# Prefix counts in two halves of 64 rows, and the second half of v loaded in two transfers

## The chip, the cores and the metric

The kernel runs on one core of a Trainium2 chip. The metric is device time in microseconds of one execution. A core has a matrix engine (TensorE, PE in the profile, with its weight loads as PEld), a vector engine (DVE), an activation engine (ACT), a general engine (POOL), and a sync engine (SP) that here does little but issue transfers. Operands lie in an on-chip memory of 128 partitions (rows); results of PE go to PSUM banks.

## The reference

Attention without a softmax, then two mixture-of-experts layers:

```python
scores = (1.0 / S) * np.matmul(z, z.transpose(0, 2, 1))     # z: 4 x 2496 x 64
attn = np.maximum(scores, 0.0) ** 2
x = u * np.matmul(attn, v)                                  # u, v: 4 x 2496 x 256
# first layer: rows with x @ w_skip > 0 go to expert argmax(x @ w_gate) of 8, the others stay
out[do_compute] = xc + gate_w * (np.maximum(xc @ w1[e], 0) @ w2[e])
# second layer: all rows, expert argmax(x @ w_gate + modality_bias[modality_id])
out[mask] = gate_w[mask, None] * (np.maximum(x[mask] @ w1[e], 0) @ w2[e])
```

Inputs are float32. 9984 rows pass through.

## The kernel before, in words

Attention runs in 20 chunks `g` of 512 query columns (448 in the last of each batch), five chunks for each of four batches. Within a chunk, 20 key blocks `k` of 128 rows go by in ten pairs `p`. For a block PE makes scores (`scores`, L1469) in a PSUM bank `pS`, ACT applies relu (L725) and square (L734) into a ring of four buffers `A`, DVE splits the square into a high part `AH` (L1118) and a low part `AL` (L1120), and PE sums `v` times these parts into `pO` (`half_sums`, L1480, and `tail_sums`, L1489), three products for each half of the 256 columns. Scores run three pairs ahead of the sums. All these matrix products are done on 64 rows of the array at a time: two matmuls, one on rows 0 to 63 and one on rows 64 to 127 (`halves`), go out as a pair and write to different banks.

`v` comes in halves of ten blocks. SP loads it into `vraw` (`load_v`, L323), which has room for ten blocks, so the second half may only be loaded over blocks that are split already. The split into `VH` is done by DVE in batch 0 (`v_high`, L1104, in the places that `V_AT`, L1123, gives), by ACT in the later batches (L708); the split into `VL` is done by POOL (`v_low`, L551). Five splits of two blocks each belong to a half. PE waits for `vl_ready` before it sums a pair.

While chunk `g` runs, the finished chunk `g-1` is routed. At p = 3 PE transposes half of its rows and computes the gate logits (`route`); at p = 7 it transposes the other half (`route_rows`, L1532, again as pairs of 64 rows, into `pT` and `pM`) and counts how many rows before each row go to each of 16 groups (`prefixes`, L1559): one matmul of the one-hot table `oh` with the triangle `before` (L1562) and four with `ones` (L1564), in bf16, on all 128 rows. DVE picks the experts (`pick_experts`) and at p = 2 of the next chunk turns the counts into destinations (`place_rows`, L1079), which wait for nothing but `prefix_ready` and ACT's copy of the rows. POOL then scatters the rows to memory by an indirect transfer for each 128 rows (L548).

All orders are written out in the code; each engine runs its list from front to back, and semaphores tie them. After chunk 20 comes a seam: the last two chunks must be placed and scattered before SP may load the first tile `xin` of the first expert layer. The two expert layers follow, which the change leaves alone. Each small DVE step that reads the result of the one before it waits for it (`step`); `ROUTE` is the number of such steps in a chunk.

Of the kernel before, what the change touches and what calls it, by code (L numbers as in the profile page):

```python
# [10 lines left out]
ALU = mybir.AluOpType  # L11
# [4 lines left out]
P = 128  # L16
# [4 lines left out]
KT = -(-S // P)  # L21
# [3 lines left out]
QT = 4  # L25
QW = QT * P
QC = KT // QT
CHUNKS = B * QC
NG = KT // QT
VU = KT // 2  # L30
# [6 lines left out]
ZW = KT * P  # L37
VW = KT * D
VHALF = KT // 2
WP = 4  # L40
GR = 2 * E
TT = 256
# [15 lines left out]
STORED = 64  # L58
MIDDLE = (3, 4, 5, 6, 8)
SPLIT_AT = ((B - 1) * QC + 1, (B - 1) * QC + 2)  # L60
ROUTE = 15


def bass_attention_two_moe(nc, u, v, z, w_skip, w_gate, w1, w2, modality, w_gate2, bias2, w2t, out):
    xs = nc.dram_tensor("token_rows", (GR * CAP + SPARE, ROW), F32, kind="Internal").ap()

    with ExitStack() as ctx:
# [6 lines left out]
        def sem(name):  # L74
            return ctx.enter_context(nc.semaphore(name))
# [83 lines left out]
        pM = pb("pM", [P, 512])  # L159
        prefix = pM[:, 2 * P:2 * P + (QT + 1) * GR].rearrange("p (t n) -> p t n", n=GR)  # L160

        xt_halves = [x[:, 0:2 * KD * H].rearrange("p (t k c) -> p t k c", t=2, k=KD) for x in (pT, pM)]

        stage1 = raw[:, 0:KD * F].rearrange("p (k f) -> p k f", k=KD)
# [37 lines left out]
        v_first_loaded = [sem(f"v_first_loaded{i}") for i in range(2)]  # L202
        z_loaded = [sem(f"z_loaded{i}") for i in range(len(Z_PARTS))]
        v_loaded = sem("v_loaded")
        u_loaded = sem("u_loaded")
        zh_ready = sem("zh_ready")
        zl_ready = sem("zl_ready")
# [104 lines left out]
        def _(sp):  # L312
            with nc.allow_non_contiguous_dma(reason="small tables"):
# [9 lines left out]
                def load_v(b, k0, k1):  # L323

                    vb = v[b, :, :]
                    full, at = min(k1, KT - 1), k0 % VHALF
                    to = vraw[:, at * D:(at + full - k0) * D].rearrange("p (j d) -> p j d", d=D)
                    sp.dma_start(to, vb[k0 * P:full * P, :].rearrange("(j p) d -> p j d", p=P)).then_inc(v_loaded if k0 >= FIRST else v_first_loaded[k0 * 2 // FIRST], 16)
                    if k1 == KT:
                        for r in range(2):  # L330
                            sp.dma_start(vraw[r * H:(r + 1) * H, (VHALF - 1) * D:VHALF * D], vb[full * P:S, :]).then_inc(v_loaded, 16)

# [3 lines left out]
                load_v(0, FIRST // 2, FIRST)  # L336
                load_z(0, 2)
                load_v(0, FIRST, VHALF)
                sp.wait_ge(vl_ready, VU // 2)
                load_v(0, VHALF, KT)  # L340
                sp.wait_ge(zeroed, 1)
                sp.dma_start(wg[:, :, 0:E], w_gate.rearrange("(k p) e -> p k e", p=P)).then_inc(consts_loaded, 16)
                sp.dma_start(wg[:, :, E:E + 1], w_skip.rearrange("(k p o) -> p k o", p=P, o=1)).then_inc(consts_loaded, 16)
# [18 lines left out]
                for b in range(B):  # L362
                    for c in range(QC):
                        load_u(b * QC + c)
                        if c == 0 and b < B - 1:
                            sp.wait_ge(zl_ready, NG * b + NG)
                            sp.wait_ge(vl_ready, VU * b + VU)
                            for part in range(len(Z_PARTS)):
                                load_z(b + 1, part)
                            load_v(b + 1, 0, FIRST // 2)  # L370
                            load_v(b + 1, FIRST // 2, FIRST)
                            load_v(b + 1, FIRST, VHALF)
                        if c == 2 and b < B - 1:
                            sp.wait_ge(vl_ready, VU * b + VU + VU // 2)
                            load_v(b + 1, VHALF, KT)

                for ph in range(2):
                    q = PH[ph]
# [277 lines left out]
        def _(act):  # L656
# [51 lines left out]
            def v_high(b, n):  # L708

                at = 2 * (n % (VU // 2)) * D  # L710
                to = (b % 2) * VW + 2 * n * D
                if 2 * n < FIRST:
                    act.wait_ge(v_first_loaded[n], 16 * b + 16)
                else:
                    act.wait_ge(v_loaded, 64 * b + (16 if 2 * n < VHALF else 64))
                s_.copy(VH[:, to:to + 2 * D], vraw[:, at:at + 2 * D]).then_inc(vh_ready, 1)
# [254 lines left out]
        def _(dve):  # L971
# [107 lines left out]
            def place_rows(idx):  # L1079
# [8 lines left out]
                dve.wait_ge(prefix_ready, idx)  # L1088
                if idx < CHUNKS:
                    dve.wait_ge(xrow_copied, 2 * idx + 2)  # L1090
                step(v_.tensor_tensor(rank[:, :, :], prefix[:, 0:QT, :], base[:, None, :].to_broadcast([P, QT, GR]), ALU.add))
                v_.tensor_tensor(base[:, :], prefix[:, QT, :], base[:, :], ALU.add).then_inc(base_ready, 1)
                step(v_.tensor_tensor(rank[:, :, :], rank[:, :, :], oh[:, 0:QT, :], ALU.mult))
                step(v_.tensor_reduce(dest_f[:, :], rank[:, :, :], AX.X, ALU.add))
                if idx > 1:
# [8 lines left out]
            def v_high(n):  # L1104
                w, at = slice(2 * n * D, 2 * (n + 1) * D), 2 * (n % (VU // 2)) * D
                if 2 * n < FIRST:
                    dve.wait_ge(v_first_loaded[n], 16)
                else:
                    dve.wait_ge(v_loaded, 16 if 2 * n < VHALF else 64)
                v_.tensor_copy(VH[:, w], vraw[:, at:at + 2 * D]).then_inc(vh_ready, 1)  # L1110
# [9 lines left out]
                    v_.tensor_tensor(AL[k % NBUF][:, 0:n], A[k % NA][:, 0:n], AH[k % NBUF][:, 0:n].bitcast(F32),  # L1120
                                     ALU.subtract).then_inc(al_ready, 1)

            V_AT = {0: (1,), 1: (2, 3), 2: (4,), 5: (5, 6), 6: (7,), 7: (8,), 8: (9,)}  # L1123
            final_done = [0]

            def f(ins):
# [319 lines left out]
        def _(pe):  # L1446
# [112 lines left out]
            def prefixes(idx):  # L1559

                pe.wait_ge(onehot_ready, idx)
                t_.matmul(pM[:, 2 * P:2 * P + (QT + 1) * GR], before[:, :], oh[:, :, :].rearrange("p t g -> p (t g)"), start=True, stop=False)  # L1562
                for i in range(QT):
                    last = t_.matmul(prefix[:, i + 1:QT + 1, :], ones[:, :], oh[:, i:i + 1, :].to_broadcast([P, QT - i, GR]),  # L1564
                                     start=False, stop=(i == QT - 1))
                last.then_inc(prefix_ready, 1)

            def scores_of(g, p):
# [285 lines left out]
```

## Time and profile before

| | |
|---|---|
| Median of three runs | 1489.77 us (1489.64 to 1490.29) |
| The profiled execution | 1489.09 us, of which the span from the first to the last instruction is 1487.2 us |
| PE busy | 1464.6 us, 98% of the span |
| DVE, ACT, POOL busy | 1009.1, 779.3, 399.2 us |
| Attention, first chunk to seam | about 11 to 704 us of the span |
| Granted TensorE clock, mean | 0.996 |

Times in rows are microseconds from the start of the span. A matrix operation's duration is longer than the distance to the next one, since they are pipelined: what a stream of them costs is read from the distance of the starts. A busy PE is therefore not a PE at its peak: time in which it empties before a change of form counts as busy.

### The profile page before, as it was taken

Reading aid. Unit: us, or ns where it says so; the run is one execution under the profiler, and the core shown is the slowest. Engines: PE = TensorE matmul, PEld = TensorE weight load, DVE = VectorE, ACT = ScalarE, POOL = GpSimd, SP = SyncE. Lnnn points to the kernel's source line nnn. Section 1 sums busy time; section 2 is a strip of 40 time slices with the busy share of each in tenths; the row PEclk is TensorE's granted clock in tenths of the full one; section 3 lists DMA queues with packets and bytes.
Section 4 is the critical chain, followed back from the end, with each engine's and each line's share of the span. In section 5 each row is a group of like instructions: output and inputs, shape, how many; then the busy total and the mean of one; then the engine's idle time right before and its main releaser. Section 6 shows DMA issues by size and latency. Waiting matters only on the chain.

```text
span 1487.2 us, 34548 instructions
## 1 busy us (share of the span) xinstructions
PE 1464.6 (98%) x11853; PEld 1279.1 (86%) x11853; DVE 1009.1 (68%) x2377; ACT 779.3 (52%) x1542; POOL 399.2 (27%) x379
## 2 busy tenths in 40 slices
PE   8999999999999999999899999999999999999997
PEld 7888988888888898888899999998888888888885
DVE  7989987999889998987666666665333343333332
ACT  6677766777667766765344444444333333333332
POOL 4133322334224332323222222224121221211212
PEclk9999999999999999999999999999999999999999
DMA  5311030211302020021533354322211121111110
GB/s 121 100 40 56 29 101 29 66 43 53 92 31 66 29 87 29 30 87 65 180 104 127 121 192 133 106 97 94 90 44 44 43 69 46 43 44 43 58 44 26
DMA packets 58009, 107.74 MB, mean 72 GB/s; under 512 B 18007, under 2 KB 32354, under 8 KB 57884
## 3 DMA queue, kind: packets, MB, share of 16 engines
q0 software_dynamic: 18464, 58.68, 11.3%
q1 hardware_dynamic: 39420, 47.48, 11.1%
q8 instruction: 68, 1.11, 0.3%
q14 instruction: 57, 0.47, 0.1%
HBM read 75.63 MB, written 32.04 MB: 72 GB/s over the span
## 4 chain that ended last, share of the span: by engine, by line
PE 95%; DMA 1%; issue 1%; DVE 1%; POOL 0%; SPq 0%; ACT 0%; POOLq 0%; ACTq 0%; DVEq 0%
PE pO L1480 33%; PE pS L1737 11%; PE pO L1745 10%; PE pS L1469 9%; PE pO L1680 9%; PE pS L1697 9%; PE pO L1747 5%; PE pM L1737 4%; PE pT L1728 1%; PE pO L1489 1%; PE pT L1627 1%; PE pM L1547 1%; PE pT L1532 1%; PE pO L1609 1%; DMA raw<-in_v_dram 0%
## 5 line engine op out<-in xcount | busy, mean ns | idle before, releaser
L1120 DVE TENSOR_TENSOR AL<-A,AH 128x512 fp32r<-128x512 f32 (+1 forms) x400 | 313.5, 784 | 13.7
L1480 PE MATMUL pO<-AH,VH 64*128 64x512 f32 (+1 forms) x1520 | 297.9, 383 | 2.6 <-POOL VL L555 1.3
L1480 PE MATMUL pO<-AL,VH 64*128 64x512 f32 (+1 forms) x1520 | 297.2, 382 | 0.0
L1480 PE MATMUL pO<-AH,VL 64*128 64x512 f32 (+1 forms) x1520 | 296.8, 381 | 0.0
L725 ACT ACTIVATE R<-pS 128x512 f32<-128x512 f32 (+1 forms) x400 | 213.4, 588 | 157.7 <-PE pS L1469 157.4
L734 ACT ACTIVATE A<-R 128x512 f32<-128x512 f32 (+1 forms) x400 | 229.7, 624 | 11.1 <-DVE AL L1120 10.9
L1118 DVE CAST AH<-A 128x512 fp32r<-128x512 f32 (+1 forms) x400 | 212.9, 532 | 30.9 <-ACT A L734 30.6
L1745 PE MATMUL pO<-VL,AH 128*128 128x512 f32 x640 | 232.2, 400 | 0.0
L1378 DVE SCALAR_TENSOR_TENSOR AL<-pS,AH 128x512 fp32r<-128x512 f32 x120 | 83.0, 692 | 157.2 <-ACT AH L896 157.1
L1747 PE MATMUL pO<-VL,AL 128*128 128x256 f32 x640 | 179.2, 280 | 0.0
L609 POOL DMA_INDIRECT out_dram<-xrow,tok_at x80 | 77.8, 973 | 365.4 <-DVE xrow L1388 352.9
L1480 PEld LDWEIGHTS pO<-AH,VH 64*128 64x128 f32 x1520 | 146.7, 184 | 28.5 <-issue 2.9
L1480 PEld LDWEIGHTS pO<-AL,VH 64*128 64x128 f32 x1520 | 146.8, 184 | 24.3
L1480 PEld LDWEIGHTS pO<-AH,VL 64*128 64x128 f32 x1520 | 146.8, 184 | 23.7
L1737 PE MATMUL pS<-ZH,VH 128*128 (+1 forms) x480 | 161.7, 391 | 0.3 <-issue 0.3
L896 ACT ACTIVATE AH<-pS 128x512 fp32r<-128x512 f32 x120 | 71.7, 598 | 171.0 <-PE pS L1737 170.8
L1745 PEld LDWEIGHTS pO<-VL,AH 128*128 128x128 f32 x640 | 120.2, 188 | 26.4
L567 POOL TENSOR_TENSOR xT<-xT,uT 128x512 f32<-128x512 f32 x38 | 50.2, 1325 | 301.7 <-DVE xT L1021 301.4
L1680 PE MATMUL pO<-ZH,VH 128*128 x736 | 128.3, 286 | 0.5 <-issue 0.5
L1747 PEld LDWEIGHTS pO<-VL,AL 128*128 128x128 f32 x640 | 120.5, 188 | 2.4
L1697 PE MATMUL pS<-VL,AH 128*128 128x264 f32 x736 | 120.8, 286 | 0.0
L855 ACT ACTIVATE AH<-pO 128x512 fp32r<-128x512 f32 x92 | 52.6, 598 | 118.7 <-PE pO L1680 118.7
(249 smaller groups left out, 2493.6 us busy)
## 6 DMA issues: line engine op xcount, KB each, us to landing
raw<-in_w_dram POOLq DMA_DIRECT2D x22, 1024.0 KB, 7.7
A<-token_rows SPq DMA_DIRECT2D x21, 536.0 KB, 3.5
uT<-in_u_dram SPq DMA_DIRECT2D x16, 512.0 KB, 3.7
xin<-token_rows SPq DMA_DIRECT2D x24, 268.0 KB, 3.0
raw<-in_v_dram SPq DMA_DIRECT2D x4, 1152.0 KB, 5.8
A<-in_w2t_dram POOLq DMA_DIRECT2D x8, 512.0 KB, 4.8
raw<-in_v_dram SPq DMA_DIRECT2D x4, 768.0 KB, 7.3
raw<-in_z_dram SPq DMA_DIRECT2D x8, 368.0 KB, 5.0
```

Of the source, the lines that this page charges most:

```text
L725: s_.activation(R[k % 2][:, 0:n], pS[k % 2][:, 0:n], ACT.Relu, scale=1.0 / S).then_inc(relu_done, 1)
L734: s_.activation(A[k % NA][:, 0:n], R[k % 2][:, 0:n], ACT.Square).then_inc(square_done, 1)
L1118: v_.tensor_copy(AH[k % NBUF][:, 0:n], A[k % NA][:, 0:n]).then_inc(ah_ready, 1)
L1120: v_.tensor_tensor(AL[k % NBUF][:, 0:n], A[k % NA][:, 0:n], AH[k % NBUF][:, 0:n].bitcast(F32), ALU.subtract).then_inc(al_ready, 1)
L1378: v_.scalar_tensor_tensor(out=AL[f][:, :], in0=ring[f % RING][:, :], scalar=0.0, in1=AH[f][:, :].bitcast(F32), op0=ALU.max, op1=ALU.subtra ...
L1469: last = t_.matmul(pS[r][:, 0:n], w[rows, (2 * p + r) * P:(2 * p + r + 1) * P], x[rows, zc:zc + n], start=(m == 0), stop=(m == 2))
L1480: last = t_.matmul(pO[:, (KD * r + d) * QW:(KD * r + d) * QW + n], vv[rows, vo + k * D + d * P:vo + k * D + (d + 1) * P], a[k % NBUF][rows ...
L1680: last = t_.matmul(pO[:, bank * 512 + fi * TT:bank * 512 + (fi + 1) * TT], w[h][:, kd, f * P:(f + 1) * P], x[:, ds(par, 1), kd, :].rearran ...
L1697: last = t_.matmul(pS[s][:, 0:width], a[p][:, fi * TT + s * P:fi * TT + (s + 1) * P], w[h][:, f, 0:width], start=(f == 0 and n == 0), stop ...
L1737: last = t_.matmul(ring[f % RING][:, :], w[h][:, kd, f * P:(f + 1) * P], x[:, ds(par, 1), kd, :].rearrange("p o t -> p (o t)"), start=(n = ...
L1745: t_.matmul(pO[:, s * QW:(s + 1) * QW].rearrange("p (m d) -> p m d", m=2), AH[f][:, rows], w2hl[h][:, :, f, 0:D], start=(f == 0), stop=(f ...
L1747: return t_.matmul(pO[:, s * QW:s * QW + D], AL[f][:, rows], w2h[h][:, f, 0:D], start=False, stop=(f == NF - 1), skip_group_check=True)
```

## The change

`prefixes` is done for chunks 1 to 19 as two halves: for rows 0 to 63 into a part of `pT`, for rows 64 to 127 into the same part of `pM`, ten matmuls of 64 rows in place of five of 128. `place_rows` adds both halves, with two more DVE instructions, each a waited step. The last routing (idx 20), after the attention, stays whole. Apart from that, the second half of `v` is loaded as six blocks (10 to 15), which wait for three `VL` splits, and then the other four, which wait for five; a semaphore of their own tells of the six. DVE's splits of v blocks from pair 5 on stand one pair earlier in its list.

```diff
+VMID = VHALF + 6
-ROUTE = 15
+ROUTE = 17
...
+        prefix_halves = [x[:, 2 * P:2 * P + (QT + 1) * GR].rearrange("p (t n) -> p t n", n=GR) for x in (pT, pM)]
...
+                sp.wait_ge(vl_ready, (VMID - VHALF) // 2)
+                load_v(0, VHALF, VMID)
                 sp.wait_ge(vl_ready, VU // 2)
-                load_v(0, VHALF, KT)
+                load_v(0, VMID, KT)
...
                         if c == 2 and b < B - 1:
+                            sp.wait_ge(vl_ready, VU * b + VU + (VMID - VHALF) // 2)
+                            load_v(b + 1, VHALF, VMID)
                             sp.wait_ge(vl_ready, VU * b + VU + VU // 2)
-                            load_v(b + 1, VHALF, KT)
+                            load_v(b + 1, VMID, KT)
...
+                parts = prefix_halves if idx < CHUNKS else [prefix]
+                step(v_.tensor_tensor(rank[:, :, :], parts[0][:, 0:QT, :], base[:, None, :].to_broadcast([P, QT, GR]), ALU.add))
+                if idx < CHUNKS:
+                    step(v_.tensor_tensor(base[:, :], parts[0][:, QT, :], base[:, :], ALU.add))
+                    step(v_.tensor_tensor(rank[:, :, :], parts[1][:, 0:QT, :], rank[:, :, :], ALU.add))
+                v_.tensor_tensor(base[:, :], parts[-1][:, QT, :], base[:, :], ALU.add).then_inc(base_ready, 1)
...
+                elif VHALF <= 2 * n < VMID:
+                    dve.wait_ge(v_mid_loaded, 16)
...
-            V_AT = {0: (1,), 1: (2, 3), 2: (4,), 5: (5, 6), 6: (7,), 7: (8,), 8: (9,)}
+            V_AT = {0: (1,), 1: (2, 3), 2: (4,), 4: (5,), 5: (6, 7), 6: (8,), 7: (9,)}
...
+                parts = list(zip(prefix_halves, halves)) if idx < CHUNKS else whole
+                for to, rows in parts:
+                    t_.matmul(to, before[rows, :], oh[rows, :, :], start=True, stop=False)
                 for i in range(QT):
+                    for to, rows in parts:
+                        last = t_.matmul(to[:, i + 1:QT + 1, :], ones[rows, :], oh[rows, i:i + 1, :].to_broadcast([P // len(parts), QT - i, GR]),
+                                         start=False, stop=(i == QT - 1))
```

PE's list at p = 7 of a chunk, before: the last transposes (L1532), the five matmuls of the count, the next scores (L1469).

```order
L1532 MATMUL pT<-ident,xT 128x64
L1532 MATMUL pM<-ident,xT 128x64
L1562 MATMUL pM<-oh,before 128x80 [waits onehot_ready]
L1564 MATMUL pM<-oh,ones 128x64
L1564 MATMUL pM<-oh,ones 128x48
L1564 MATMUL pM<-oh,ones 128x32
L1564 MATMUL pM<-oh,ones 128x16
L1469 MATMUL pS<-ZH 128x512 [waits relu_done]
```

The same place in the changed kernel, where these lines are L1548, L1581, L1584 and L1485:

```order
L1548 MATMUL pT<-ident,xT 128x64
L1548 MATMUL pM<-ident,xT 128x64
L1581 MATMUL pT<-oh,before 128x80 [waits onehot_ready]
L1581 MATMUL pM<-oh,before 128x80
L1584 MATMUL pT<-oh,ones 128x64
L1584 MATMUL pM<-oh,ones 128x64
L1584 MATMUL pT<-oh,ones 128x48
L1584 MATMUL pM<-oh,ones 128x48
L1584 MATMUL pT<-oh,ones 128x32
L1584 MATMUL pM<-oh,ones 128x32
L1584 MATMUL pT<-oh,ones 128x16
L1584 MATMUL pM<-oh,ones 128x16
```

Each count matmul has become two, one for each half of the rows, side by side like the transposes ahead of them.

DVE's list in chunk 0 from pair 5 on, before (L1118 and L1120 split a block of squares, L1110 two blocks of v):

```order
L1102 TENSOR_TENSOR ZL<-raw,ZH 128x512 [waits zh_ready]
L1118 CAST AH<-A 128x512 [waits pv_done,square_done]
L1120 TENSOR_TENSOR AL<-A,AH 128x512 [waits ah_ready]
L1118 CAST AH<-A 128x512 [waits pv_done,square_done]
L1120 TENSOR_TENSOR AL<-A,AH 128x512 [waits ah_ready]
L1110 CAST VH<-raw 128x512 [waits v_loaded] x2
```

And now (L1134, L1136, L1126):

```order
L1116 TENSOR_TENSOR ZL<-raw,ZH 128x512 [waits zh_ready]
L1126 CAST VH<-raw 128x512 [waits v_mid_loaded]
L1134 CAST AH<-A 128x512 [waits pv_done,square_done]
L1136 TENSOR_TENSOR AL<-A,AH 128x512 [waits ah_ready]
L1134 CAST AH<-A 128x512 [waits pv_done,square_done]
L1136 TENSOR_TENSOR AL<-A,AH 128x512 [waits ah_ready]
L1126 CAST VH<-raw 128x512 [waits v_mid_loaded] x2
```

One v split has moved ahead of the two square splits, and the next two wait for the six-block transfer alone.

DVE's destinations for a chunk, before:

```order
L1091 TENSOR_TENSOR rank<-pM,base 128x64 [waits xrow_copied,prefix_ready]
L1092 TENSOR_TENSOR base<-pM,base 128x16 [waits route_step]
L1093 TENSOR_TENSOR rank<-rank,oh 128x64
L1094 TENSOR_REDUCE dest_f<-rank 128x4 [waits route_step]
L1097 TENSOR_TENSOR dest<-dest_f,invalid 128x4 [waits route_step]
```

And now:

```order
L1102 TENSOR_TENSOR rank<-pT,base 128x64 [waits xrow_copied,prefix_ready]
L1104 TENSOR_TENSOR base<-pT,base 128x16 [waits route_step]
L1105 TENSOR_TENSOR rank<-pM,rank 128x64 [waits route_step]
L1106 TENSOR_TENSOR base<-pM,base 128x16 [waits route_step]
L1107 TENSOR_TENSOR rank<-rank,oh 128x64
L1108 TENSOR_REDUCE dest_f<-rank 128x4 [waits route_step]
L1111 TENSOR_TENSOR dest<-dest_f,invalid 128x4 [waits route_step]
```

Two instructions are added, and two more of them wait for the one ahead.

## Rows read from the trace of the kernel before

**Rows 1.** The page, part 1: busy time, share, instructions of each engine.
```profile
PE 1464.6 (98%) x11853; PEld 1279.1 (86%) x11853; DVE 1009.1 (68%) x2377; ACT 779.3 (52%) x1542; POOL 399.2 (27%) x379
```

**Rows 2.** Waits of PE: line, releaser, us in total, times, longest.
```profile
PE pT L1627 <- DMA xin<-token_rows: 4.6, 1, 4.6
...
PE pO L1480 <- POOL VL L555: 1.3, 1, 1.3
PE pO L1480 <- DVE xT L1021: 1.2, 1, 1.2
```

**Rows 3.** Timeline of PE at the count: start, us, line, operation, [idle].
```profile
113.91 0.21 PE L1532 MATMUL pT<-ident,xT 64*128 64x64 f32 x1
...
114.09 0.22 PE L1532 MATMUL pT<-ident,xT 64*128 64x64 f32 x1
114.09 0.22 PE L1532 MATMUL pM<-ident,xT 64*128 64x64 f32 x1
114.24 0.21 PE L1562 MATMUL pM<-oh,before 128*128 128x80 bf16 x1
114.28 0.26 PE L1564 MATMUL pM<-oh,ones 128*128 128x64 bf16 x4
114.47 0.50 PE L1469 MATMUL pS<-ZH 64*128 64x512 f32 x2
114.81 0.40 PE L1469 MATMUL pS<-ZL,ZH 64*128 64x512 f32 x2
115.04 0.39 PE L1469 MATMUL pS<-ZH,ZL 64*128 64x512 f32 x2
```

**Rows 4.** Instructions of tile pM, 113.8 to 114.6: duration ns min/median/max.
```profile
L1532 PEld LDWEIGHTS pM<-ident,xT x4: 135/138/140, 113.7 to 114.0; 64*128 64x128 f32 x4
...
L1564 PEld LDWEIGHTS pM<-oh,ones x4: 96/98/105, 114.3 to 114.3; 128*128 128x128 bf16 x4
L1564 PE MATMUL pM<-oh,ones x4: 169/182/200, 114.3 to 114.4; 128*128 128x64 bf16 x1, 128*128 128x48 bf16 x1, 128*128 128x32 bf16 x1, 128*128 128x16 bf16 x1
```

**Rows 5.** Chain of waits, 20 to 66 us: start, us, what.
```profile
24.63 6.10 DMA raw<-in_v_dram
...
31.36 1.29 POOL VL L555
...
50.17 0.69 DVE xT L1021
...
51.00 3.02 PE pO L1480 x24
```

**Rows 6.** Timeline of DVE in chunk 0.
```profile
30.75 0.76 DVE L1110 CAST VH<-raw 128x512 fp32r<-128x512 f32 x2 [0.76 <-DMA raw<-in_v_dram]
...
32.95 1.67 DVE L1120 TENSOR_TENSOR AL<-A,AH 128x512 fp32r<-128x512 f32 x1
```

**Rows 7.** Timeline of POOL in chunk 0.
```profile
16.74 2.73 POOL L555 TENSOR_TENSOR VL<-raw,VH 128x512 fp32r<-128x512 f32 x2 [2.74 <-DVE VH L1110]
```

**Rows 8.** Timeline of DVE at the seam.
```profile
700.30 0.23 DVE L1091 TENSOR_TENSOR rank<-pM,base 128x64 f32<-128x64 f32 x1 [0.86 <-ACT xkeep L687]
700.56 0.17 DVE L1092 TENSOR_TENSOR base<-pM,base 128x16 f32<-128x16 f32 x1
700.65 0.21 DVE L1093 TENSOR_TENSOR rank<-rank,oh 128x64 f32<-128x64 f32 x1
...
703.53 0.69 DVE L1203 TENSOR_TENSOR xT<-xT,uT 128x512 f32<-128x512 f32 x1
```

**Rows 9.** Timeline of POOL at the seam.
```profile
702.42 1.02 POOL L548 DMA_INDIRECT token_rows<-xkeep,dest  x1 [1.18 <-issue]
703.74 1.36 POOL L548 DMA_INDIRECT token_rows<-xkeep,dest  x1 [0.30 <-issue]
```

**Rows 10.** Timeline of DVE near the end of chunk 3.
```profile
150.74 0.69 DVE L1120 TENSOR_TENSOR AL<-A,AH 128x512 fp32r<-128x512 f32 x1
```

**Rows 11.** Timeline of PE at the same place.
```profile
153.02 0.40 PE L1489 MATMUL pO<-AH,VH 64*128 64x512 f32 x2
```

More of the change, by code:

```diff
@@ L204, in bass_attention_two_moe @@
         v_loaded = sem("v_loaded")
+        v_mid_loaded = sem("v_mid_loaded")
         u_loaded = sem("u_loaded")
@@ L326, in load_v @@
                     full, at = min(k1, KT - 1), k0 % VHALF
+                    done = v_first_loaded[k0 * 2 // FIRST] if k0 < FIRST else v_mid_loaded if k0 == VHALF else v_loaded
                     to = vraw[:, at * D:(at + full - k0) * D].rearrange("p (j d) -> p j d", d=D)
-                    sp.dma_start(to, vb[k0 * P:full * P, :].rearrange("(j p) d -> p j d", p=P)).then_inc(v_loaded if k0 >= FIRST else v_first_loaded[k0 * 2 // FIRST], 16)
+                    sp.dma_start(to, vb[k0 * P:full * P, :].rearrange("(j p) d -> p j d", p=P)).then_inc(done, 16)
                     if k1 == KT:
@@ L713, in v_high @@
                     act.wait_ge(v_first_loaded[n], 16 * b + 16)
+                elif VHALF <= 2 * n < VMID:
+                    act.wait_ge(v_mid_loaded, 16 * b + 16)
                 else:
@@ L1090, in place_rows @@
                     dve.wait_ge(xrow_copied, 2 * idx + 2)
-                step(v_.tensor_tensor(rank[:, :, :], prefix[:, 0:QT, :], base[:, None, :].to_broadcast([P, QT, GR]), ALU.add))
-                v_.tensor_tensor(base[:, :], prefix[:, QT, :], base[:, :], ALU.add).then_inc(base_ready, 1)
+                parts = prefix_halves if idx < CHUNKS else [prefix]
[4 more added lines that the diff above has]
+                v_.tensor_tensor(base[:, :], parts[-1][:, QT, :], base[:, :], ALU.add).then_inc(base_ready, 1)
                 step(v_.tensor_tensor(rank[:, :, :], rank[:, :, :], oh[:, 0:QT, :], ALU.mult))
@@ L1107, in v_high @@
                     dve.wait_ge(v_first_loaded[n], 16)
+                elif VHALF <= 2 * n < VMID:
+                    dve.wait_ge(v_mid_loaded, 16)
                 else:
@@ L1561, in prefixes @@
                 pe.wait_ge(onehot_ready, idx)
-                t_.matmul(pM[:, 2 * P:2 * P + (QT + 1) * GR], before[:, :], oh[:, :, :].rearrange("p t g -> p (t g)"), start=True, stop=False)
+                whole = [(prefix, slice(0, P))]
+                parts = list(zip(prefix_halves, halves)) if idx < CHUNKS else whole
+                for to, rows in parts:
+                    t_.matmul(to, before[rows, :], oh[rows, :, :], start=True, stop=False)
                 for i in range(QT):
-                    last = t_.matmul(prefix[:, i + 1:QT + 1, :], ones[:, :], oh[:, i:i + 1, :].to_broadcast([P, QT - i, GR]),
-                                     start=False, stop=(i == QT - 1))
+                    for to, rows in parts:
+                        last = t_.matmul(to[:, i + 1:QT + 1, :], ones[rows, :], oh[rows, i:i + 1, :].to_broadcast([P // len(parts), QT - i, GR]),
+                                         start=False, stop=(i == QT - 1))
                 last.then_inc(prefix_ready, 1)
```

## The prediction

> **What bounds the kernel now.** I read the page first. PE is busy for 98% of the span [rows 1], no other engine for more than 68%, so PE's list sets the time and only what shortens or stops that list counts. Next the waits of PE: in all of attention and the seam behind it three are longer than a microsecond [rows 2], and two of those lie in the places that the change touches: 1.3 us for the low part of v (POOL, L555) in chunk 0, and 4.6 us at the seam for the first tile of the first expert layer. The third, 1.2 us on DVE's L1021 between chunks 0 and 1, is where the gain of the first will be cut. A busy PE can still lose time when it changes its form, so last I read the timeline of PE around the count [rows 3]; the distances between starts are what the stream costs.
>
> **Part 1: the count in halves (chunks 1 to 19).** The rows to compare are the starts in [rows 3]. The four pairs of transposes start from 113.91 to 114.09, 0.06 apart; then 0.15 pass until the count's first matmul, the five matmuls start 0.03 to 0.04 apart (the last of four L1564 ends 0.26 after the first starts and the shortest last 0.17, so it starts 0.09 after it, at about 114.37), 0.10 pass until the first scores, and their second pair comes 0.34 after the first, where the next distance is 0.23 [rows 3, 4]. So the count spends its time less on its matmuls than on going from 64 rows to 128 and back. From the last transposes to the second pair of scores it is 114.81 - 114.09 = 0.72 us.
>
> In the changed kernel this stretch holds one form throughout. Bounds of what it then takes:
> - Best: a pair costs what one matmul of the same width costs. 0.06 (the transposes' own distance) + 0.04 + 0.09 for the five pairs + 0.04 to the scores + 0.23 = 0.46, a gain of 0.26 a chunk.
> - Middle: a pair costs 0.06 like a pair of transposes. 0.06 + 5 x 0.06 + 0.23 = 0.59, a gain of 0.13.
> - Worst of these: the middle, and the first scores keep their extra 0.11 (0.34 against 0.23). 0.70, a gain of 0.02.
>
> Which? The two halves of one pair of transposes start together (114.09 twice), so a second half next to the first costs under 0.01. And the transposes' 0.06 looks like their weight load: its record lasts 138 ns in fp32, that of the bf16 count 98 [rows 4]. Both speak for the best end; I take 0.21, closer to it. The Trainium skill (TensorEngine Tiling (Array Packing), Key Properties) says that changing the tiling mode drains the engine, which is what the 0.15 and the 0.10 look like.
>
> A rule of the Trainium skill speaks against this part: TensorE: Matmul & The Clock Gate, in "Wait — 56ns, not 53.3ns?", puts the start-to-start distance at no less than about 25 ns however few columns a matmul has, and five matmuls are added. If that held across the halves too, 5 x 25 ns = 0.13 of an estimated gain of 0.26 would go. The pair at 114.09 does not bear it out for matmuls in different halves; the rival below works the case from rows.
>
> Chunk 19's exit lies ahead of a wait of 4.6 us and gains nothing, so 18 chunks count: 18 x 0.21 = 3.8 us. Nothing stretches in between: ACT's copies and the scores three pairs ahead follow PE's own times.
>
> **Part 2: two more steps on DVE.** At the seam the first rank step starts at 700.30, the base step 0.26 later and the next 0.09 behind that [rows 8]. A waited step costs its duration and 0.03. The new list is rank 0.26, base 0.17 + 0.03 = 0.20, rank 0.26, base 0.09: 0.81 against 0.35, so 0.46 us more a chunk. In chunks 1 to 18 they run at p = 2 of the next chunk, beside PE's sums. What is late next would be AL. The tightest place I found is the last block of chunk 3: AL is finished at 150.74 + 0.69 = 151.43, PE takes it at 153.02 [rows 10, 11], 1.6 us later. 0.46 fits in even if none of it is caught up. Cost: nothing.
>
> At the seam it is on the path: the counts of chunk 19, ACT's copies, `place_rows`, POOL's four indirect transfers, the load of `xin`, PE. The halves give back 0.09 ahead of it (0.15 to 0.06), so the scatter would begin 0.37 later. But the second indirect issue lasts 1.36 against 1.02 for the first, and starts while DVE multiplies two on-chip operands at L1203 (703.53 to 704.22) [rows 8, 9]. That multiply hangs on PE's sums, which come 0.2 earlier, while the scatter comes 0.37 later; the second issue then starts behind it and loses its 0.34. Bounds: -0.1, if a later issue escapes a multiply as well, to +0.46, if none does and the halves give nothing back. I take 0.
>
> **Part 3: v in two transfers.** The whole second half is loaded only when five VL splits are done; it starts at 24.63 and takes 6.10 [rows 5], and DVE stands still for 0.76 before its L1110 at 30.75 [rows 6]. POOL's first split of that half runs from 31.36 to 32.65 [rows 5], and PE has waited 1.3. Now the six blocks need three splits. POOL's third is the first of the two at 16.74, done at 18.1 [rows 7]. The SP has nothing else to issue then. The nine blocks took 6.10 [rows 5]; if six take no less, they are there at about 25. DVE was through with pair 5 at 30.0 (30.75 - 0.76) and its two blocks take some 1.1 each, so the moved L1110 comes at 27.8: no wait. POOL is done with it at about 29.6 (1.3 for the split, and some 0.4 until it starts), and PE wants it at 31.3 (32.65 less its wait). So the 1.3 us wait goes, whole.
>
> Not all of that stays. From 31 to 50 us DVE never stops: the L1021 at 50.17 follows its splits directly, and PE goes on at 51.00 behind the first of two [rows 5]. All its work in chunk 0 is the same in the changed kernel; only the 0.76 of idle goes. Each L555 on POOL stretches a DVE operation beside it (1.67 instead of 0.69 [rows 6, 10]), and with five of them in either order that is unchanged too. So L1021 starts 0.76 earlier and PE with it; PE meets DVE a little earlier, in short waits for AL or for scores' banks in pairs 6 to 9. Gain 0.76. Bounds: 0.3, if one more VL split stretches DVE by half of its 1.0, to 1.3, if nothing binds. In the later batches ACT splits v long before PE needs it, and PE shows no wait there: nothing.
>
> **Sum.** -3.8 + 0 - 0.8 = -4.6. Made against the profiled execution, 1489.1 (1487.2 of span and 1.9 around it), it gives 1484.5. That execution lies 0.7 below the median of the runs, 1489.8; from the median it is 1485.2, which I give.
>
> **Rivals.**
> 1. *The second half of each pair costs a start of its own.* For it: the narrow matmuls at L1564 come no closer than 0.03, though the last have a quarter of the columns of the first [rows 3]. Against it: the pairs of transposes. Ten starts at 0.03 are 0.30, the middle bound: 0.13 x 18 + 0.8 = 3.1, so 1486.7; with the extra 0.11 left it is 0.4 + 0.8 = 1.2, so 1488.6.
> 2. *The gaps are not the change of form* but the change from fp32 to bf16 and back, and the halves do not remove them. For it: in these rows both change at once. Then five pairs in place of five matmuls change nothing, and only chunk 0 gains, less the seam: -0.8 + 0.4, 1489.4.
> 3. *DVE does not bind in chunk 0*, and PE keeps the 1.3: 0.5 us more, 1484.7. Against it: L1021 right behind the splits.
> 4. *Slower: the halves run one after another*, each paying its own weight load like a transposes pair. Ten times 0.06 + 0.06 + 0.10 + 0.34 = 1.10 in place of 0.72: +0.38 x 18 = 6.8, with the other parts +6.4, 1496.2. It decides from where an added matmul costs over 0.05 (0.26 / 5). Against it: equal starts at 114.09.
>
> **How the numbers follow.** The forecast, gains of 0.17 to 0.26 a chunk, has 0.53, rival 3 with it 0.07, rival 1 0.25, rival 2 0.11, rival 4 0.04. Two parts in a thousand, 3.0 us, is about what a measurement of this kernel can tell from no change; the border is 1486.8. Faster by more: all of the forecast and rival 3, and a part (0.09) of rival 1: 0.69. Slower by more: rival 4, and 0.01 for what I did not see: 0.05. The rest, 0.26, is the same. The range: 0.26 x 18 + 1.3 + 0.1 = 6.1 gives 1483.7 at the low end; at the high end 1488.6 takes in rival 1 whole and leaves rivals 2 and 4.
>
> **What would show it.** In the changed profile: the count's first pair starts 0.06 behind the last transposes, five pairs 0.03 to 0.04 apart, and the scores' second pair 0.23 behind their first, so that the 0.72 becomes about 0.5. The wait on L555 is gone from PE's list and L1021 of chunk 1 starts at about 49.4. At the seam the load of `xin` starts as long after the last count as before. I am wrong if the stretch of 0.72 shrinks by less than 0.15, if new waits of PE on AL appear past chunk 0, or if the wait at the seam has grown by more than 0.4.

## The result: slower by about 2 us

The changed kernel takes 1492.28 us in the median of 18 runs (1491.37 to 1493.27), the kernel before 1489.95 us in 18 runs beside it. The ratio is 1.0015, 95% interval 1.0008 to 1.0021. The forecast was 1485.2 us, its range 1483.7 to 1488.6. The prediction gave 0.26 to a time less than 3.0 us from the kernel before, where this one lies, on the slower side (+2.3 us; the interval is 1.2 to 3.1), and 0.05 to a slower time beyond that. The profiled execution took 1491.7 us, its span 1490.1; its mean granted clock is 0.996, as before. The clock differs in one place, behind the attention: from the first transposes of `xin` to the first sums of the expert layer it is 0.63 before and 0.75 now, and that stretch takes 7.26 against 6.18 us. The rest of the span behind it is 1.2 us longer, so it plays no part in the loss.

The page, part 1, against [rows 1]: DVE is busy 12.9 us longer, with 38 instructions more (19 chunks times two); PE is busy 2.0 us less, in a span that is 2.9 longer.

```profile
PE 1462.6 (98%) x11948; PEld 1288.2 (86%) x11948; DVE 1022.0 (69%) x2415; ACT 781.9 (52%) x1542; POOL 398.1 (27%) x379
```

The waits of PE, against [rows 2]:

```profile
PE pO L1496 <- DVE xT L1031: 5.5, 10, 0.9
PE pT L1647 <- DMA xin<-token_rows: 4.6, 1, 4.6
```

The wait for the low part of v is gone and the seam's is the same. The wait on the addition of the finished sum row to `xT` (L1031, before L1021) was one of 1.2 us; now there are ten with 5.5 us in all, and nine of them, 5.2 us, lie beyond chunk 0. They are the loss.

The timeline of PE at the count (here chunk 1's; start, us, line, operation), against [rows 3]:

```profile
78.03 0.22 PE L1548 MATMUL pT<-ident,xT 64*128 64x64 f32 x1
...
78.09 0.20 PE L1581 MATMUL pT<-oh,before 64*128 64x80 bf16 x1
78.09 0.20 PE L1581 MATMUL pM<-oh,before 64*128 64x80 bf16 x1
78.12 0.19 PE L1584 MATMUL pT<-oh,ones 64*128 64x64 bf16 x1
...
78.21 0.17 PE L1584 MATMUL pT<-oh,ones 64*128 64x16 bf16 x1
...
78.23 0.48 PE L1485 MATMUL pS<-ZH 64*128 64x512 f32 x2
78.55 0.39 PE L1485 MATMUL pS<-ZL,ZH 64*128 64x512 f32 x2
```

From the last transposes to the second pair of scores it is 78.55 - 78.03 = 0.52 us in place of 0.72. So PE's own list did become shorter, by the forecast 0.2 a chunk.

The distance from one count to the next, in us, read from the starts of its first matmul in the timelines of PE, shows where it is given back. The columns "at" are starts themselves; under 2 stands the distance from count 1 to count 2, and so on:

| kernel | count 1 at | 2 | 3 | 4 | 5 | 6 | 7 | count 19 at | 20 at |
|---|---|---|---|---|---|---|---|---|---|
| before | 79.04 | 35.20 | 35.15 | 32.28 | 35.05 | 35.17 | 35.17 | 699.14 | 710.01 |
| changed | 78.09 | 34.98 | 35.81 | 33.15 | 35.38 | 34.97 | 34.97 | 702.02 | 712.78 |

The same three distances are longer in batches 1 and 2 (8 to 10: +0.61, +0.88, +0.41; 13 to 15: +0.61, +1.15, +0.13), 5.65 us in all with the first three; the other nine from 2 to 19 are 1.82 shorter; ahead of the first it is 0.95: -0.95 - 1.82 + 5.65 = 2.88, the distance at count 19.

Why these three? The work of each engine in a stretch of the kernel before (the stretch and its length, then us busy and instructions of PE, its weight loads, DVE, ACT and POOL), from 0.05 us behind one count to the same point behind the next:

```profile
79.09:114.29 35.20, 35.20 (x335) 28.71 (x334) 30.87 (x62) 26.13 (x52) 13.14 (x11) 1.00 0.21 69
114.29:149.45 35.16, 35.16 (x335) 28.71 (x334) 33.38 (x67) 25.91 (x52) 13.38 (x11) 1.00 0.10 33
216.78:251.96 35.18, 35.18 (x335) 28.71 (x334) 27.89 (x67) 23.34 (x47) 6.71 (x6) 1.00 0.09 30
```

The third sum is DVE's: 33.38 us in the stretch that ends at count 3, 27.89 in the one that ends at count 6. DVE has 68% of the whole span but 95% there, and 94 and 90% in the two stretches that follow (30.42 of 32.28 and 31.62 of 35.05 us); this the share of the whole span hides. What fills the list is above all POOL's splitting of the next v: four L555 in a row, beside which one conversion of DVE lasts 5.67 us (timelines of POOL and DVE, kernel before). The same four stand at 97.35, ahead of the first of the three additions that come late; ahead of the third it is three splits of `z`.

```profile
132.62 5.03 POOL L555 TENSOR_TENSOR VL<-raw,VH 128x512 fp32r<-128x512 f32 x4
```
```profile
132.28 5.67 DVE L1118 CAST AH<-A 128x512 fp32r<-128x512 f32 x1
```

The start of the chunk that follows count 2, in DVE's timeline of the kernel before, with POOL's and PE's behind it:

```profile
120.34 0.68 DVE L1021 TENSOR_TENSOR xT<-pO,xT 128x512 f32<-128x512 f32 x1
121.64 0.69 DVE L1021 TENSOR_TENSOR xT<-pO,xT 128x512 f32<-128x512 f32 x1 [0.62 <-ACT xT L671]
122.25 0.54 DVE L1118 CAST AH<-A 128x512 fp32r<-128x512 f32 x1
122.82 1.67 DVE L1120 TENSOR_TENSOR AL<-A,AH 128x512 fp32r<-128x512 f32 x1
...
125.47 0.22 DVE L1091 TENSOR_TENSOR rank<-pM,base 128x64 f32<-128x64 f32 x1
...
126.40 0.43 DVE L1118 CAST AH<-A 128x512 fp32r<-128x512 f32 x1
```
```profile
121.20 2.74 POOL L567 TENSOR_TENSOR xT<-xT,uT 128x512 f32<-128x512 f32 x2 [12.39 <-DVE xT L1021]
```
```profile
121.50 0.39 PE L1480 MATMUL pO<-AH,VH 64*128 64x512 f32 x2
```

and of the changed one, likewise:

```profile
120.12 1.28 DVE L1031 TENSOR_TENSOR xT<-pO,xT 128x512 f32<-128x512 f32 x2
121.31 1.24 DVE L1134 CAST AH<-A 128x512 fp32r<-128x512 f32 x1
122.59 1.67 DVE L1136 TENSOR_TENSOR AL<-A,AH 128x512 fp32r<-128x512 f32 x1
...
125.24 0.22 DVE L1102 TENSOR_TENSOR rank<-pT,base 128x64 f32<-128x64 f32 x1
...
126.64 0.42 DVE L1134 CAST AH<-A 128x512 fp32r<-128x512 f32 x1
...
142.47 1.82 DVE L1136 TENSOR_TENSOR AL<-A,AH 128x512 fp32r<-128x512 f32 x1
```
```profile
120.98 2.74 POOL L575 TENSOR_TENSOR xT<-xT,uT 128x512 f32<-128x512 f32 x2 [13.34 <-DVE xT L1031]
```
```profile
120.95 0.50 PE L1496 MATMUL pO<-AH,VH 64*128 64x512 f32 x2 [0.57 <-DVE xT L1031]
```

PE may not overwrite the sum row in `pO` before DVE has read it: in the changed kernel it goes on 0.15 us after the end of the first addition (120.12 + 0.68 = 120.80). Before, its first sums came at 121.50, 0.48 after the addition's end (121.02). That is a slack of some 0.33 us; at the start of the next chunk it was the same and at the third none. In the changed kernel the distance is 0.15 at all nine, which is no slack.

From this addition to the next chunk's, DVE took 34.86 us before (120.34 to 155.20) and 35.70 after (120.12 to 155.82). Of the 0.84, the steps that place the counts are 0.46 (125.47 to 126.40 before, 125.24 to 126.64 after: 0.93 against 1.40, as forecast). The conversion behind the additions is 0.70 longer: POOL's two multiplications (L567, now L575) begin when the first addition is done. Before, the conversion started 1.05 us behind them and took 0.54; with no idle time of DVE between the additions it starts 0.33 behind them and takes 1.24. A further 0.38 comes from a v split of POOL near 142 us, which stretches a subtraction (1.82) where before it met a small copy (L1045, 0.93). And 0.70 is won, since the second addition no longer starts late, behind ACT's copy: 0.46 + 0.70 + 0.38 - 0.70 = 0.84.

### The profile page after: what moved, and what is told of

The parts are those of the page before. It is cut to its first block, busy times and chain, and to the rows that moved or that the text cites. A ratio compares the mean times of both kernels' runs of the same rounds, so it can differ in the third digit from the quotient of the medians.

```text
span 1490.1 us, 34780 instructions
## 1 busy us (share of the span) xinstructions
PE 1462.6 (98%) x11948; PEld 1288.2 (86%) x11948; DVE 1022.0 (69%) x2415; ACT 781.9 (52%) x1542; POOL 398.1 (27%) x379
## 3 DMA queue, kind: packets, MB, share of 16 engines
HBM read 75.63 MB, written 32.04 MB: 72 GB/s over the span
## 4 chain that ended last, share of the span: by engine, by line
PE 85%; DVE 7%; issue 6%; DMA 1%; ACT 1%; POOL 0%; POOLq 0%; SPq 0%; ACTq 0%; DVEq 0%
PE pO L1496 26%; PE pS L1757 11%; PE pO L1765 10%; PE pO L1700 9%; PE pS L1717 9%; PE pS L1485 7%; PE pO L1767 5%; DVE AH L1134 4%; PE pM L1757 3%; PE pT L1748 1%; DVE AL L1136 1%; PE pT L1647 1%; PE pO L1505 1%; PE pM L1563 1%; PE pO L1629 1%
## 5 line engine op out<-in xcount | busy, mean ns | idle before, releaser
L1136 DVE TENSOR_TENSOR AL<-A,AH 128x512 fp32r<-128x512 f32 (+1 forms) x400 | 322.5, 806 | 13.7
L1496 PE MATMUL pO<-AH,VH 64*128 64x512 f32 (+1 forms) x1520 | 305.0, 384 | 6.0 <-DVE xT L1031 5.5
L1496 PE MATMUL pO<-AL,VH 64*128 64x512 f32 (+1 forms) x1520 | 304.3, 382 | 0.0
L1496 PE MATMUL pO<-AH,VL 64*128 64x512 f32 (+1 forms) x1520 | 303.8, 382 | 0.0
L1134 DVE CAST AH<-A 128x512 fp32r<-128x512 f32 (+1 forms) x400 | 219.1, 548 | 25.3 <-ACT A L744 25.1
L1496 PEld LDWEIGHTS pO<-AH,VH 64*128 64x128 f32 x1520 | 152.9, 184 | 31.7 <-issue 9.5
L1496 PEld LDWEIGHTS pO<-AL,VH 64*128 64x128 f32 x1520 | 153.3, 184 | 20.7
L1496 PEld LDWEIGHTS pO<-AH,VL 64*128 64x128 f32 x1520 | 153.2, 184 | 20.4
L575 POOL TENSOR_TENSOR xT<-xT,uT 128x512 f32<-128x512 f32 x38 | 50.6, 1342 | 303.7 <-DVE xT L1031 303.7
```

The costliest lines, as they stand in the source:

```text
L1134: v_.tensor_copy(AH[k % NBUF][:, 0:n], A[k % NA][:, 0:n]).then_inc(ah_ready, 1)
L1496: last = t_.matmul(pO[:, (KD * r + d) * QW:(KD * r + d) * QW + n], vv[rows, vo + k * D + d * P:vo + k * D + (d + 1) * P], a[k % NBUF][rows ...
```

## The experiments

Each ran beside the kernel before; changes are shown against that kernel or the changed one, as said. The times of the kernel before in the three groups of runs were 1489.93, 1490.77 and 1490.35 us.

**Each part alone**, against the kernel before. First the v transfers and DVE's earlier v splits, with the count whole:

```diff
+VMID = VHALF + 6
...
+                sp.wait_ge(vl_ready, (VMID - VHALF) // 2)
+                load_v(0, VHALF, VMID)
                 sp.wait_ge(vl_ready, VU // 2)
-                load_v(0, VHALF, KT)
+                load_v(0, VMID, KT)
```

> The v transfers and the earlier v splits alone, with the count as before. Theory A (DVE's two added steps make its L1021, the sum of the halves of pO, late in the chunks in which it is loaded most): this part is innocent, 0.9 us faster than before (1489.0), all of it in chunk 0, no wait of PE on the sum rows in later chunks. Rival B (the extra transfer of v in batches 1 to 3 disturbs): at least 2 us slower than before, with waits from chunk 2 on. Rival C (PE's earlier arrival moves POOL's work onto DVE's): as A here.

Measured: 1489.44 us, ratio 0.9998 (0.9989 to 1.0007). Count 1 comes at 78.44 and PE has no later wait for `xT`; count 19 comes 0.52 earlier than before. A gain of this size lies below what the measurement tells.

Then the halves and their steps, with v in one transfer:

```diff
-ROUTE = 15
+ROUTE = 17
...
+                parts = list(zip(prefix_halves, halves)) if idx < CHUNKS else whole
```

> The count in halves and its two added DVE steps alone, v loaded as before. A: slower than before by what the change lost and v had hidden, 2.3 + 0.9 = 3.2 us, so 1493.2; waits of PE on the sum rows at the start of chunks 3, 4 and 5 of each of the first three batches, chunks 0.2 shorter elsewhere. B: 2 to 4 us faster than before. C: as A.

Measured: 1492.5 us, ratio 1.0016 (1.0007 to 1.0025). Ten waits for `xT`, 6.4 us, of which 1.2 in chunk 0 as in the kernel before. So the halves with their steps are the slower part, whole.

**The steps alone.** The kernel before, PE's list untouched, with two waited steps of the same shapes, which read PSUM too and write to a spare tile:

```diff
+                if idx < CHUNKS:
+                    step(v_.tensor_tensor(spare[:, QT, :], prefix[:, QT, :], base[:, :], ALU.add))
+                    step(v_.tensor_tensor(spare[:, 0:QT, :], prefix[:, 0:QT, :], rank[:, :, :], ALU.add))
```

> The kernel before with two more DVE steps per chunk of the same shapes at the same place, which write a tile that nobody reads; the count on PE is unchanged, so PE gets no faster. A: slower than before by 2 to 5 us, by 0.1 to 0.9 in each of the nine loaded chunks, nothing elsewhere, since L1021 has only 0 to 0.3 us to spare there. B: no change. C: no change within 0.5 us, since PE comes no earlier.

Measured: 1494.39 us, ratio 1.0035 (1.0021 to 1.0049). Its waits of PE:

```profile
PE pO L1484 <- DVE xT L1022: 4.6, 9, 1.2
```

Of these 4.6 us 1.2 are the one wait of chunk 0 that was there before. The loaded distances are 35.78, 33.10, 35.36, those of the changed kernel (35.81, 33.15, 35.38), with all others within 0.05 of the kernel before. This isolates the cause: two steps of together 0.46 us on DVE cost 4.5 us of the whole. With the halves added (the run ahead of this one) the way from count 1 to count 19 is 2.1 us shorter (623.70 against 625.78), which is the nine unloaded distances at some 0.23; in the loaded ones PE's gain only becomes a longer wait.

**The additions earlier.** If DVE is late at the start of a chunk, take the first addition ahead of the last block of squares:

```diff
+                    if g > 0 and k == 2:
+                        sum_rows(g, 0).then_inc(o_summed, 1)
...
-                            add_sums(g)
+                            sum_rows(g, 1).then_inc(o_summed, 1)
```

> The changed kernel with the first of the two sum-row additions one block of squares earlier in DVE's list (between the second and the third block of the new chunk's first four, about 1.1 us earlier). A: PE's waits on the sum rows go, 5 to 6 us faster than the changed kernel, 1486.5, faster than before too. If POOL's earlier multiply collides with DVE as a result, half of that. B and C: within 1 us of the changed kernel.

Measured: 1497.32 us, ratio 1.0050 (1.0037 to 1.0064). The expectation was wrong. DVE's timeline, then POOL's and PE's:

```profile
119.43 0.68 DVE L1031 TENSOR_TENSOR xT<-pO,xT 128x512 f32<-128x512 f32 x1
...
120.48 1.67 DVE L1136 TENSOR_TENSOR AL<-A,AH 128x512 fp32r<-128x512 f32 x1
122.08 0.68 DVE L1031 TENSOR_TENSOR xT<-pO,xT 128x512 f32<-128x512 f32 x1
...
123.12 1.67 DVE L1136 TENSOR_TENSOR AL<-A,AH 128x512 fp32r<-128x512 f32 x1
```
```profile
120.30 1.31 POOL L575 TENSOR_TENSOR xT<-xT,uT 128x512 f32<-128x512 f32 x1 [12.27 <-DVE xT L1031]
122.93 1.32 POOL L575 TENSOR_TENSOR xT<-xT,uT 128x512 f32<-128x512 f32 x1 [1.33 <-DVE xT L1031]
```
```profile
122.81 0.50 PE L1498 MATMUL pO<-AH,VH 64*128 64x512 f32 x2 [0.89 <-DVE xT L1031]
```

POOL's two multiplications, apart now, each stretch a subtraction, and the first delays the second addition, for which PE now waits. The unloaded chunks get longer too (35.25 where 34.97 stood). So what lies beside POOL's multiplications is worth as much as when DVE gets to the addition.

**Halves where DVE has room.** The nine counts that DVE places ahead of the late additions (1 to 3, 6 to 8, 11 to 13) stay whole:

```diff
+        def in_halves(idx):
+            return idx < CHUNKS and (idx > (B - 1) * QC - 2 or idx % QC in (0, QC - 1))
```

> The changed kernel with the count in halves only for idx 4, 5, 9, 10 and 14 to 19; for the nine others, whose destinations DVE works out in the chunks in which it is loaded most, the count is whole and the two added steps are gone. A (in those nine chunks DVE's list sets the chunk's length, in the others PE's): loaded chunks back to 35.15, 32.1 and 35.1 us, the ten with halves 0.2 shorter, v's 0.6 in chunk 0: 1487.3, faster than before and 5 us faster than the changed kernel. Rival D (each added step costs PE wherever it stands): the ten chunks gain nothing, 1489.4 or more.

Measured: 1488.53 us, ratio 0.9989 (0.9980 to 0.9998). That is 2.2 us faster than the kernel before; 1487.3 us was expected. The first two loaded distances are back at 35.20 and 32.07, the waits for `xT` are two with 0.5 us. The third is not back: 35.68, and 35.40 and 35.15 in batches 1 and 2, where 35.1 was expected. Of its excess in batch 0, 0.23 us comes at the sum row (187.71) and 0.49 at the gate logits near 202 us, where the profile shows no releaser; the cause of that part stays open.

**One step fewer.** Both halves are added at 80 columns in two steps, and `base` is copied from the sum:

```diff
+                    step(v_.tensor_tensor(both[:, :, :], prefix_halves[0], base[:, None, :].to_broadcast([P, QT + 1, GR]), ALU.add))
+                    step(v_.tensor_tensor(both[:, :, :], prefix_halves[1], both[:, :, :], ALU.add))
+                    v_.tensor_copy(base[:, :], both[:, QT, :]).then_inc(base_ready, 1)
```

> The changed kernel with its two halves added over all five columns of the table at once, and the base copied from the result: one added waited step (0.25 us) in place of two (0.46). A: the loaded chunks lose about half as much (35.5 in place of 35.78), 1.5 to 2 us faster than the changed kernel, 1490.5. If only the number of POOL and DVE meetings counts and not the length of the steps: within 0.5 us of the changed kernel.

Measured: 1490.3 us, ratio 0.9998 (0.9989 to 1.0007); loaded distances 35.28, 32.94, 35.28, six waits with 2.6 us. Half of the added DVE time costs about half.

**The steps between the additions.** DVE idles there 0.62 us for ACT's copy in the kernel before. The changed kernel with its count steps moved there:

```diff
-                            add_sums(g)
+                            sum_rows(g, 0).then_inc(o_summed, 1)
+                            if g > 1:
+                                place_counts(g - 1)
+                            sum_rows(g, 1).then_inc(o_summed, 1)
```

> The changed kernel with the first four steps of the destinations (up to the new base) moved from p = 2 to between the two sum-row additions, where DVE stood idle for 0.6 us in the kernel before and where POOL's first multiply finds it reading PSUM. A: DVE has 0.5 to 1.2 us more in each loaded chunk, PE's waits on the first sum rows go, 1486.5. If PE then waits for the second sum rows instead, as it did with the earlier first addition: 0.3 us in each of 18 chunks, 1490 or more.

Measured: 1486.8 us, ratio 0.9974 (0.9963 to 0.9984). DVE's timeline:

```profile
119.53 0.69 DVE L1031 TENSOR_TENSOR xT<-pO,xT 128x512 f32<-128x512 f32 x1
120.13 0.21 DVE L1102 TENSOR_TENSOR rank<-pT,base 128x64 f32<-128x64 f32 x1
...
120.94 0.68 DVE L1031 TENSOR_TENSOR xT<-pO,xT 128x512 f32<-128x512 f32 x1
121.54 0.44 DVE L1149 CAST AH<-A 128x512 fp32r<-128x512 f32 x1
122.01 1.67 DVE L1151 TENSOR_TENSOR AL<-A,AH 128x512 fp32r<-128x512 f32 x1
```

The steps fill the gap, and only one instruction is stretched. The first distances are 34.98, 34.95, 32.04, 35.09, 34.97.

**The same move without the halves**, with the v transfers:

```diff
+                parts = [prefix]
...
+                            sum_rows(g, 0).then_inc(o_summed, 1)
+                            if g > 1:
+                                place_counts(g - 1)
```

> The v transfers alone, with the whole count's two steps moved between the two sum-row additions in the same way; no halves. A: PE was bound by nothing there after the start, so as v alone, 1489.4, up to 0.3 faster. If the place between the additions costs PE a wait: slower by 1 us or more.

Measured: 1489.72 us, ratio 0.9996 (0.9987 to 1.0005). Where DVE is not late the move gains nothing; the halves are worth 2.9 us on top of it (1489.72 to 1486.8).

**The move with the steps alone**, against the kernel before: the two spare steps, and all count steps between the additions.

```diff
+            def place_counts(idx):
...
+                    step(v_.tensor_tensor(spare[:, QT, :], prefix[:, QT, :], base[:, :], ALU.add))
+                    step(v_.tensor_tensor(spare[:, 0:QT, :], prefix[:, 0:QT, :], rank[:, :, :], ALU.add))
```

> The kernel before with the same two added steps of DVE as in the run that adds only them (1494.4 us), and all the steps that place the counts between the two additions of the sum row; nothing of PE's is changed. Theory A (it is where the steps lie in DVE's list that decides): they cost nothing or little, 1489.5 to 1491 us, and the chunks at the start of a batch are back within 0.2 us of the kernel before. Theory B (their length in a full list decides wherever they lie): 1493 to 1494 us, with PE waiting for the sum row in nine chunks.

Measured: 1489.37 us, ratio 0.9993 (0.9984 to 1.0002), against 1.0035 with the same steps in their old place. The first four distances are those of the kernel before, within 0.01. The steps' length alone isn't what costs; their place is.

**The move with a step fewer** joins the two edits, `both` and the place between the additions:

```diff
+                    v_.tensor_copy(base[:, :], both[:, QT, :]).then_inc(base_ready, 1)
...
+                            if g > 1:
+                                place_counts(g - 1)
```

> The changed kernel with the steps that place the counts between the two additions of the sum row, and the two additions of the halves of the count made one step. Theory A (DVE's idle time between the additions takes up to about 0.7 us of steps for nothing): with a step less, what is left between the additions is shorter still, the few waits of PE for the sum row go, 1486.3 to 1486.8 us. Theory B (a wait on another row is next): the same as with two additions there, 1486.8 us.

Measured: 1491.66 us, ratio 1.0006 (0.9997 to 1.0015), a miss: 4.9 us more than without the merging. PE waits twelve times for `xT`, 3.7 us, and the loaded distances are 35.46, 32.63 and 35.80. (The traced execution took 1489.95 us, 1.7 less than the median.) DVE's timeline, then POOL's:

```profile
119.67 0.23 DVE L1103 TENSOR_TENSOR both<-pT,base 128x80 f32<-128x80 f32 x1
119.94 0.24 DVE L1104 TENSOR_TENSOR both<-pM,both 128x80 f32<-128x80 f32 x1
120.22 1.04 DVE L1105 COPY base<-both 128x16 f32<-128x16 f32 x1
121.17 0.68 DVE L1032 TENSOR_TENSOR xT<-pO,xT 128x512 f32<-128x512 f32 x1
```
```profile
119.94 1.29 POOL L576 TENSOR_TENSOR xT<-xT,uT 128x512 f32<-128x512 f32 x1 [12.40 <-DVE xT L1032]
122.03 1.31 POOL L576 TENSOR_TENSOR xT<-xT,uT 128x512 f32<-128x512 f32 x1 [0.81 <-DVE xT L1032]
```

A copy of 16 columns, on-chip to on-chip, stands 1.04 us beside POOL's multiplication (0.17 in its old place), delays the second addition and with it POOL, which stretches the next subtraction as well. The four steps that read PSUM kept their 0.21, 0.17, 0.23 and 0.17 in the same place.

**The steps behind the additions**, where DVE has no idle time, but POOL's multiplications run:

```diff
                             add_sums(g)
+                            if g > 1:
+                                place_counts(g - 1)
...
-                            place_rows(g - 1)
+                            place_dest(g - 1)
```

> The changed kernel with all the steps that place the counts put right behind both additions of the sum row, ahead of the next chunk's first conversion, so that DVE does the same work as in the changed kernel but its steps that read PSUM lie beside POOL's two multiplications. Theory A (what costs is mostly that the first conversion now meets POOL's multiplications and takes 1.24 us instead of 0.54): the conversion goes back to about 0.54 us, the chunk at the start of a batch loses up to 0.7 us of its 0.85, most waits of PE for the sum row go, and the time is 1487 to 1488.5 us. Theory B (what costs is only that the added steps are more work in a DVE list that is full in these chunks): the waits stay as in the changed kernel, and the time is about 1492 us.

Measured: 1486.91 us, ratio 0.9977 (0.9967 to 0.9987). DVE's timeline, then POOL's:

```profile
121.61 0.17 DVE L1106 TENSOR_TENSOR base<-pM,base 128x16 f32<-128x16 f32 x1
121.70 1.32 DVE L1149 CAST AH<-A 128x512 fp32r<-128x512 f32 x1
123.05 0.69 DVE L1151 TENSOR_TENSOR AL<-A,AH 128x512 fp32r<-128x512 f32 x1
```
```profile
120.18 2.55 POOL L575 TENSOR_TENSOR xT<-xT,uT 128x512 f32<-128x512 f32 x2 [12.40 <-DVE xT L1031]
```

The time is what theory A said, its mechanism only in part: the conversion did not go back to 0.54, it is still stretched (1.32), but the subtraction behind it is not (0.69 in place of 1.67), since POOL is done at 122.73. One collision of two is gone, about 0.9 us a chunk. Theory B, that DVE's amount of work alone decides, falls: its instructions are those of the changed kernel. This and the move between the additions beat both kernels, by 3.4 to 4.0 us against the kernel before.

## Why the prediction was wrong, step by step

- *Part 1, the count in halves.* The mechanism and the size were right: pairs start 0.03 apart, entry 0.06, exit 0.02, gain 0.20 against 0.21 taken. Only the scores' first distance kept 0.32 where I expected 0.23. The rows also settle the rivals on this part: a second half costs no start of its own (rivals 1 and 4), and the passages shrink although the type still changes (rival 2). The gain does not add up over 18 chunks, because in nine of them PE is not what binds once DVE has been lengthened.
- *Part 2, "Cost: nothing".* This is the step that failed. I looked for what is late next, took AL alone, and found 1.6 us at the end of chunk 3 [rows 10, 11]. Behind chunk 0 AL was never late. But DVE's list is one row, and at the start of the next chunk PE needs another thing of it, the addition of the sum row; there the slack was 0.33, 0.33 and 0. "If new waits of PE on AL appear" named the wrong tile; the waits came on `xT`. With PE's list untouched the term measures +0.63, +0.82 and +0.31 in the loaded distances of the first batch (35.78, 33.10, 35.36 against 35.15, 32.28, 35.05), and 4.5 us in the whole; in the changed kernel the nine are 5.65 longer where 9 x 0.21 = 1.9 shorter was forecast.
- *Part 2, the 0.46 itself* was right to the hundredth, but as a price it was short: the steps took away the DVE idle time that kept the conversion clear of POOL. Two things work together, a full list and a collision more: with the steps behind the additions DVE's work is the same and one collision less, and the loaded distances are 35.06, 32.30 and 35.17, within 0.3 of the best seen.
- *Part 2, the seam.* The first indirect transfer starts 3.73 us behind count 19 in place of 3.28, later by 0.45 where 0.37 was forecast; the second escapes the multiply, as reasoned, and is issued in 1.00 in place of 1.36. The wait for `xin` is 4.6 as before: right.
- *Part 3, v in two transfers.* PE's wait on L555 is gone; the moved v split comes at 27.73 (27.8 forecast) and POOL is done with its part at 29.64 (29.6); DVE's first addition for chunk 1 comes at 49.30 in place of 50.17, and PE goes on at 50.13 in place of 51.00 [rows 5]: 0.87 against 0.76 taken. DVE's timeline, then PE's piece in the chain of waits, both of the changed kernel:

```profile
49.30 1.28 DVE L1031 TENSOR_TENSOR xT<-pO,xT 128x512 f32<-128x512 f32 x2
```
```profile
50.13 3.03 PE pO L1496 x24
```

The comparison holds because these two traces begin alike: ahead of any difference the same DVE subtraction stands at 22.40 and 22.36, while in two other traces with v in one transfer the v split at 21.61 of the kernel before stands at 21.27 and 22.80. In the time of the whole the gain is too small to be measured (0.9998).
- *The rivals.* All four were about PE's own matmuls or chunk 0; rival 3 fell too, since PE waits 0.3 us for the addition at the end of chunk 0. The case that came, that DVE becomes the bound of a few chunks, was not among them, though the page had a place for it: DVE's busy share in those stretches.

What stays open is the seam of the better versions. With the steps between the additions count 19 comes 3.6 us earlier than before, but count 20 only 2.2, and the distance there is 12.29 where 10.87 stood; with those behind them the 3.0 us of count 19 are all kept (10.77). Two others show it as well (12.25 with the halves where DVE has room, 12.11 with a step fewer). The longer distance is no loss in itself: in all three the wait for `xin` is shorter (2.7 to 3.2 us against 4.6), and with the steps between the additions PE begins on `xin` 4.1 us earlier than before. It is lost behind that. From there to the first sums of the expert layer this version takes 8.30 us against 6.27 with the steps behind the additions, and 2.4 us of it are four gaps of PE (713.62 to 716.52) for which the profile shows no releaser; the other two have 0.7 and 2.0 us of such gaps at the same place, the remaining traces none. What they are wasn't tested. Each kernel has one trace, and that of the version with the steps behind the additions lies 1.8 us below its median, so the difference may be one between executions and not between kernels: the medians of the two are 1486.8 and 1486.91.

## What to carry to other kernels

Before an edit on an engine that is not the bound is costed at nothing, list every thing that the bound engine takes from it (here AL, AH and the addition of the sum row), and read the slack of each at the stretch where that engine is fullest, not over the span. Where two engines hinder each other, ask what the added work displaces into the other's operations, and place it where it is not stretched: here steps that read PSUM, put beside POOL's multiplications, kept their lengths, and a copy of 16 columns took 0.87 us longer.

## What the runs showed of the hardware

- Beside a POOL operation on two on-chip tensors, DVE's conversion went from 0.42 to 1.24 or 1.32, its subtraction from 0.69 to 1.67 and a 16-column copy from 0.17 to 1.04; four POOL operations in a row held one conversion for 5.67 us. DVE's operations that read PSUM (0.17 to 0.23, and the addition of 0.68) were not stretched by them. The Trainium skill (SBUF — State Buffer, "SBUF: two separate sides") has DVE and GpSimd share one port pair as an exclusive lock, held for a whole instruction, and names as the DVE operations subject to it those with two SBUF inputs and those in a two-port mode. The trace agrees for the subtraction, which has two such inputs; the operations with one input in PSUM kept their length. It adds that DVE need not get its turn between POOL's instructions: with four ready, the conversion ended 0.30 us after the last of them (137.95 against 137.65), though its record starts 0.34 before the first; beside the two multiplications it ended (122.55) before the second did (123.72).
- Ten count matmuls of 64 rows, as pairs in different halves, start within 0.12 us (78.09 to 78.21): a pair shares one start, also in bf16.
- The passage between matmuls of 64 and of 128 rows costs some 0.09 on the way in and 0.08 on the way out (0.15 and 0.10 before against 0.06 and 0.02), and it is gone with the halves although fp32 and bf16 still alternate: it is the form and not the type.
